# An attention and two-layer feed-forward kernel on one core: value products four slots behind their scores, the first pair normalised in two token halves, the root by Newton steps on VectorE

## The reference, cut to what matters

```python
# q, k, v: (4, 8, 576, 64) float32
rel = pos[:, None] - pos[None, :]
mask = (rel >= 0) & (rel < 64)                  # causal, window of 64
scores = np.where(mask, scale * (q @ k.T), -1e9)
attn = exp(scores - max(scores)); attn = attn / (sum(attn) + 1e-9)
x = (attn @ v), as 2304 tokens x 512

rms = np.sqrt(np.mean(x * x, axis=-1, keepdims=True) + 1e-06)
xn = x / rms * rms_g                            # the normalisation
g = xn @ w_gate; h = g * sigmoid(g) * (xn @ w_val)      # 512 -> 1536
y = h @ w_out                                   # 1536 -> 512
out = (relu(y @ w_in) ** 2) @ w_out2            # 512 -> 2048 -> 512
```

## Time and profile before

| | |
|---|---|
| median of 3 runs | 879.01 us (877.69 to 879.26) |
| the profiled execution, its own time | 876.42 us |
| its span | 874.7 us |
| mean granted TensorE clock | 0.998 of full speed |
| PE busy | 854.7 us (98%) |
| PEld busy | 841.5 us (96%) |
| DVE busy | 591.4 us (68%) |
| ACT busy | 478.8 us (55%) |
| POOL busy | 466.0 us (53%) |

### The profile page before, as it was taken

How to read it: one execution, slowest core, us unless ns; L and a number is a source line. 1 busy time by engine, 2 the same in 40 slices (tenths; PEclk the granted TensorE clock), 3 DMA queues, 4 the chain that set the end, 5 groups by cost and what they waited for, 6 DMA issues and landing times.

```text
span 874.7 us, 16801 instructions
## 1 busy us (share of the span) xinstructions
PE 854.7 (98%) x6388; PEld 841.5 (96%) x6388; DVE 591.4 (68%) x728; ACT 478.8 (55%) x1005; POOL 466.0 (53%) x473
## 2 busy tenths in 40 slices
PE   7798999999999999999999999999999999999998
PEld 5687999999999999999999999999999999999998
DVE  4758675558567548755557767687577787577982
ACT  5887665545565645455555455454555454555451
POOL 3756398683589765388857368400187400386100
PEclk9999999999999999999999999999999999999999
DMA  8863122222222212222212222256632166522687
GB/s 281 263 220 87 49 73 73 61 61 61 84 73 70 70 55 61 79 73 73 73 55 64 81 67 73 56 158 228 218 87 72 56 218 184 176 73 97 182 256 237
DMA packets 107871, 100.18 MB, mean 115 GB/s; under 512 B 6928, under 2 KB 85776, under 8 KB 107792
## 3 DMA queue, kind: packets, MB, share of 16 engines
q1 hardware_dynamic: 92544, 84.14, 32.3%
q10 hardware_dynamic: 15248, 14.98, 4.9%
HBM read 79.69 MB, written 19.40 MB: 113 GB/s over the span
## 4 chain that ended last, share of the span: by engine, by line
PE 90%; DVE 5%; issue 2%; ACT 1%; DMA 1%; POOL 1%; DVEq 0%; ACTq 0%; POOLq 0%
PE banks L844 29%; PE banks L845 28%; PE banks L846 28%; PE banks L803 1%; PE banks L745 1%; DVE probsT L1488 1%; ACT probs L1159 1%; PE banks L817 1%; DMA w_kept<-stash 1%; PE banks L777 1%; DVE acts L1428 0%; DVE banks L1468 0%; DVE d_lo L1574 0%; DVE xc_lo L1460 0%; PE banks L753 0%
## 5 line engine op out<-in xcount | busy, mean ns | idle before, releaser
L844 PE MATMUL banks<-xc_hi,w_hi 128*128 128x384 f32 x844 | 282.6, 335 | 0.2 <-DVE xc_lo L1460 0.2
L846 PE MATMUL banks<-xc_hi,w_lo 128*128 128x384 f32 x844 | 281.9, 334 | 0.0
L845 PE MATMUL banks<-xc_lo,w_hi 128*128 128x384 f32 x844 | 281.9, 334 | 0.0
L844 PE MATMUL banks<-hs_hi,d_hi 128*128 128x384 f32 x544 | 182.4, 335 | 2.3 <-DVE d_lo L1574 2.2
L846 PE MATMUL banks<-hs_hi,d_lo 128*128 128x384 f32 x544 | 181.8, 334 | 0.0
L845 PE MATMUL banks<-hs_lo,d_hi 128*128 128x384 f32 x544 | 181.7, 334 | 0.0
L844 PEld LDWEIGHTS banks<-xc_hi,w_hi 128*128 128x128 f32 x844 | 158.4, 188 | 0.6 <-DVE xc_lo L1460 0.4
L845 PEld LDWEIGHTS banks<-xc_lo,w_hi 128*128 128x128 f32 x844 | 158.4, 188 | 0.0
L846 PEld LDWEIGHTS banks<-xc_hi,w_lo 128*128 128x128 f32 x844 | 158.4, 188 | 0.0
L1405 DVE TENSOR_TENSOR w_lo<-w_raw,w_hi 128x1024 fp32r<-128x1024 f32 x58 | 77.1, 1329 | 81.8 <-ACT w_hi L1090 81.8
L572 POOL TENSOR_TENSOR w_raw<-w_raw 128x256 f32<-128x256 f32 x58 | 60.8, 1047 | 134.0 <-DMA w_raw<-in_w_in 113.6
(11 more groups left out here) (114 smaller groups left out, 1342.5 us busy)
## 6 DMA issues: line engine op xcount, KB each, us to landing
w_kept<-stash SPq DMA_DIRECT2D x56, 256.0 KB, 3.1
w_raw<-in_w_gate SPq DMA_DIRECT2D x36, 256.0 KB, 2.9
w_raw<-in_w_val SPq DMA_DIRECT2D x72, 128.0 KB, 2.8
d_raw<-in_w_out SPq DMA_DIRECT2D x36, 256.0 KB, 2.6
d_raw<-in_w_down SPq DMA_DIRECT2D x32, 256.0 KB, 3.0
v_sb<-in_v_rows SPq DMA_DIRECT2D x16, 384.0 KB, 5.0
w_raw<-in_w_in SPq DMA_DIRECT2D x24, 256.0 KB, 2.7
w_raw<-in_w_in SPq DMA_DIRECT2D x48, 128.0 KB, 2.6
```

The source lines that it names most:

```text
L844: pe.matmul(ps, w_h, v_h, start=first, stop=False, skip_group_check=joined)
L845: pe.matmul(ps, w_h, v_l, start=False, stop=False, skip_group_check=joined)
L846: return pe.matmul(ps, w_l, v_h, start=False, stop=last, skip_group_check=joined)
```

## The change

`PV_LAG` becomes 4: the value products of group `g - 4` stand in slot `g`, and ACT's copies of their results with them. Slot 19 has the products of group 15 and, behind the feed-forward products, those of group 16; slot 20 those of group 17 (`values_in`, `results_in`). On POOL the scaling of the maximum (`biased`) now stands ahead of the add on the sums (`summed`). The first pair is normalised in two chains, one for each half. Per half the four squares are first added in pairs (on POOL in slot 10 for half 0, on DVE in slot 13 for half 1), so PE sums 12 matmuls instead of 24 (slots 11 and 14). The root and the reciprocal are replaced, in all three pairs, by `inverse_root`: a first guess from the bits of the number and two Newton steps, seven small instructions on DVE, each waiting for the one before. ACT takes no root any more.

```diff
-N_LAG, T_LAG, PV_LAG, O_LAG = 1, 2, 3, 3
+N_LAG, T_LAG, PV_LAG = 1, 2, 4
...
+def values_in(g):
+    return [g - PV_LAG] if PV_LAG <= g < TAIL - 1 else [GROUPS - 1] if g == TAIL - 1 else []
+def results_in(g):
+    return [GROUPS - 2, GROUPS - 1] if g == TAIL - 1 else values_in(g)
...
+            def square_two(kh, c):
+                of = x_block(0, kh, c)
+                nc.gpsimd.tensor_tensor(sq_all[:, 2 * kh:2 * kh + 2, c * NT:(c + 1) * NT], of, of,
+                                        ALU.mult).then_inc(sq_pool, 1)
...
                 if g in (8, 9):
                     pool.wait_ge(o_out, O_DONE[A_GROUP + 1])
-                    for k in (2 * (g - 8), 2 * (g - 8) + 1):
-                        square_half(k, 0)
+                    square_two(g - 8, 0)
                 if g == 10:
+                    pool.wait_ge(sq_pool, 2)
+                    nc.gpsimd.tensor_tensor(sq_all[:, 0:2, 0:NT], sq_all[:, 0:2, 0:NT], sq_all[:, 2:4, 0:NT],
+                                            ALU.add).then_inc(sq_added, 1)
+                if g == 11:
+                    first_diagonals(0)
+                if g == 12:
+                    pool.wait_ge(o_out, O_DONE[B_GROUP + 1])
+                    square_two(0, 1)
+                if g == 13:
                     high1_plain(1)
                     high2_plain(1)
-                if g == 13:
-                    diagonals(0)
                 if g == 14:
+                    first_diagonals(1)
+                if g == 15:
                     low1_plain(1)
-                if g == 15:
+                if g == 16:
                     low2_plain(1)
...
-                if g == 10:
+                if g == 11:
                     pe.wait_ge(consts, CONSTS)
-                    pe.wait_ge(sq_pool, KT)
+                    pe.wait_ge(sq_added, 1)
                     first_sums(0, bank[5])
                 if g == 12:
-                    first_sums(1, bank[5])
-                if g == 14:
-                    spread_half(0, bank[5])
+                    spread_half(0, bank[5])
+                if g == 14:
+                    pe.wait_ge(sq_added, 2)
+                    pe.wait_ge(norm_done, KT)
+                    first_sums(1, bank[5])
+                if g == 15:
                     spread_half(1, bank[5])
...
+            def inverse_root(nth, tiles):
+                done = STEPS * nth
+                m, x, e = rms[:, tiles], guess[:, tiles], resid[:, tiles]
+                dve.wait_ge(ms_done, nth + 1)
+                nc.vector.tensor_scalar(x.bitcast(I32), m.bitcast(I32), -0.5, ROOT_SEED, ALU.mult,
+                                        ALU.add).then_inc(rinv_done, 1)
+                for n, (by, plus) in enumerate(ROOT_STEPS):
+                    dve.wait_ge(rinv_done, done + 1 + 3 * n)
+                    nc.vector.tensor_tensor(e, x, x, ALU.mult).then_inc(rinv_done, 1)
...
-                if g == 12:
-                    mean_square(0, bank[5])
-                if g == 13:
-                    inverse(0)
-                if g in (14, 15):
+                if g in (11, 14):
+                    mean_square(nth, bank[5], tiles)
+                    inverse_root(nth, tiles)
+                if g in (12, 13):
...
-                    for k in (2 * (g - 14), 2 * (g - 14) + 1):
+                    for k in (2 * (g - 12), 2 * (g - 12) + 1):
                         normalise(half_cols(0, k, 0), k, bank[5][:, 0:NT])
+                if g == 13:
+                    nc.vector.tensor_tensor(sq_all[:, 0:2, NT:PW], sq_all[:, 0:2, NT:PW], sq_all[:, 2:4, NT:PW],
+                                            ALU.add).then_inc(sq_added, 1)
+                if g in (15, 16):
+                    for k in (2 * (g - 15), 2 * (g - 15) + 1):
+                        normalise(half_cols(0, k, 1), k, bank[5][:, 0:NT])
                 if g in (16, 17):
-                    x_low(0, "B11")
...
+                    x_low(0, ("B11", "B21")[g - 16])
```

More of the change, by code:

```diff
@@ L204, in build @@
         rms = sb("rms", [P, TB], F32)
+        guess = sb("guess", [P, TB], F32)
+        resid = sb("resid", [P, TB], F32)
         assert top[0] <= nc.sbuf_usable_end, (top[0], nc.sbuf_usable_end)
         T1, T2, T3, T4 = [sb(f"T{n + 1}", [P, PW], F32, temp_at + n * PW * 4) for n in range(4)]
-        squares = [[sb(f"sq{n}_{k}", [P, PW], F32, at + k * PW * 4) for k in range(KT)]
-                   for n, at in enumerate((hs_at, h_at + C1 * PW * 4))]
+        sq_all = sb("sq_all", [P, KT, PW], F32, hs_at)
+        squares = [[sq_all[:, k, :] for k in range(KT)],
+                   [sb(f"sq{k}", [P, PW], F32, h_at + (C1 + k) * PW * 4) for k in range(KT)]]
         diag = [sq[0] for sq in squares]
@@ L633, in _ @@
                 if 0 <= n < GROUPS:
+                    total = sums[:, n % PR, :]
+                    pool.wait_ge(exp_done, n + 1)
+                    nc.gpsimd.tensor_scalar(total, total, 1e-9, None, ALU.add).then_inc(summed, 1)
                     pool.wait_ge(inverted, n + 1)
@@ L815, in first_sums @@
                 for n in range(c * TB // 2, (c + 1) * TB // 2):
-                    for k in range(KT):
+                    for k in range(2):
                         mm = pe.matmul(ps[:, n:n + 1], squares[0][k][:, n * P:(n + 1) * P], ones[:, 0:1],
-                                       start=k == 0, stop=k == KT - 1)
-                if c == 1:
-                    mm.then_inc(ms_mm, 1)
+                                       start=k == 0, stop=k == 1)
+                mm.then_inc(ms_mm, 1)
             def spread_part(q, ps, n):
@@ L1162, in _ @@
                     mm.then_inc(exp_done, 1)
-                if g == B_GROUP + O_LAG:
+                if g == B_GROUP + PV_LAG:
                     act.wait_ge(o_out, O_DONE[B_GROUP + 1])
-                    square_half(2, 1)
-                    square_half(3, 1)
-                if g == 12:
-                    root(0)
-                if g in (15, 16):
-                    x_high(0, ("B11", "B21")[g - 15], KT)
+                    nc.scalar.activation(sq_all[:, 2:4, NT:PW], x_block(0, 1, 1), ACT.Square).then_inc(sq_done, 1)
+                if g in (14, 15):
+                    x_high(0, ("B11", "B21")[g - 14], KT)
                 if g in (17, 18):
@@ L1415, in low2, with mean_square @@
                                         ALU.subtract).then_inc(lo2_done, 1)
[L1417 to L1425 removed]
+            def mean_square(nth, ps, tiles):
+                dve.wait_ge(ms_mm, nth + 1)
+                nc.vector.tensor_scalar(rms[:, tiles], ps[:, tiles], 1.0 / D, 1e-6, ALU.mult, ALU.add).then_inc(ms_done, 1)
+            def inverse_root(nth, tiles):
[7 more added lines that the diff above has]
+                    nc.vector.tensor_tensor(e, x, x, ALU.mult).then_inc(rinv_done, 1)
+                    dve.wait_ge(rinv_done, done + 2 + 3 * n)
+                    nc.vector.scalar_tensor_tensor(out=e, in0=e, scalar=by, in1=m, op0=ALU.mult,
+                                                   op1=ALU.mult).then_inc(rinv_done, 1)
+                    dve.wait_ge(rinv_done, done + 3 + 3 * n)
+                    nc.vector.scalar_tensor_tensor(out=x, in0=e, scalar=plus, in1=x, op0=ALU.add,
+                                                   op1=ALU.mult).then_inc(rinv_done, 1)
             def normalise(x, k, by):
```

88 lines of the change are left out of this document (35 added, 53 removed).

## The result

| | before | after |
|---|---|---|
| median of the runs | 878.02 us (14 runs) | 881.75 us (14 runs) |
| the profiled execution, its own time | 876.42 us | 884.91 us |
| its span | 874.7 us | 883.2 us |
| mean granted TensorE clock | 0.998 | 0.986 |

The account below looks back on a forecast made before the run. DVE's slot with its round trip to POOL was taken to set the pace until PE's full stretch; -0.84 for earlier entry, +1.1 value products, +0.75 copy wait gave +1.0 on 879.01, 880.0. Range 875.8 to 883.8.

Parts of the forecast that it names:

- POOL's new order delays DVE by 0.69 us a slot: Attention slots: DVE's reciprocal waits for POOL's `summed` behind `biased`, making DVE's slot 3.31 us instead of 2.62.
- The rival that the order is free: Attention slots: POOL's order costs nothing, ACT bounds at 3.1 us up to group 10, -6.4 us, 873.6; chance 0.08.
- The chains in attention: DVE slots 11 and 14: mean and root, eight dependent instructions, 1.7 us each, 3.4 in all.
- the upper bound I leaned on: DVE's chains: upper bound of the pitch between dependent small instructions, 0.18 + 0.09 = 0.27 us; the lower was 0.13.
- DVE's extras: DVE slots 11 to 17: chains 3.4, normalising two blocks 4.2, add of squares and low part 1.74, together 9.34 us.
- PE's stalls hidden but for 0.3 us: Attention slots: lag 4 gives PE 1.05 to 1.3 us of slack, hiding its waitless stalls but 0.3 us.
- the slower rival: Slots 4 to 10: slack doesn't hide PE's stalls, +3.7 us, 883.7; decides from one stall of about 2 us; chance 0.28.
- Maximum of group 17 at 74.8: Start of DVE's last row maximum: 14.41 + 15 slots x 3.31 + 9.34 + 1.1 + 0.3 = 74.8, against 75.32 before.
- Behind the last maximum: Span after group 17's maximum: forecast 800.9 us, including +1.1 for more value products and +0.75 for ACT's copy.
- In pairs 1 and 2 the chain of seven delays `ga` by about 1.2 us: Later pairs: `va` comes behind it, hidden by two PE products; if not, two pairs lose a few tenths.
- my border of no change: Whole kernel: about 0.2%, 1.8 us, can't be told from no change, so 877.2 to 880.8 counts as same.
- The signs: Attention and after: maxima 3.3 us apart, group 11's at 45 to 46, PE's full stretch at 78.3, no waits behind 87.

Follow-up runs that it names:

- Both repairs together: Changed kernel with POOL's old order and the roots of pairs 1 and 2 at the end of step 8: 874.44 us, 0.9956 of before.
- the roots moved: Changed kernel with the seven small instructions of pairs 1 and 2 moved from the head of step 9 to the end of step 8: 879.07 us.
- after again: The changed kernel run once more, unedited, against the kernel before: 882.04 us, ratio 1.0038.
- the repaired version: Changed kernel, POOL's old order, later roots in step 8, group 16's products between the feed-forward products: 874.30 and 872.80 us; with filler matmuls 873.81.

## Why the prediction was near in time, and which steps failed

The absolute time owes something to luck: 880.0 was +1.0 us on a median of three runs, 879.01, and the kernel before has a median of 878.02 over 14. Measured is +3.4 by medians and +4.2 by the ratio. The sum had these steps; each is held against the runs.

- **POOL's new order delays DVE by 0.69 us a slot: right**, measured 0.7 to 0.8. Of its parts one was sized low: `biased` to `summed` is 0.32, not 0.26, so 15 slots cost 0.9 us more. The rival that the order is free (873.6) fell with the run that restored the old order. Both repairs together took 874.4, near that rival's number, but not by its working: it had 3.1 us a slot up to group 10, and that kernel's profile has 3.6.
- **The chains in attention: right in kind, high in size.** Eight instructions and the next one's start, 1.7 forecast:

```profile
68.24 0.15 DVE L1435 TENSOR_SCALAR rms<-banks 128x3 f32<-128x3 f32 x1
...
69.61 0.17 DVE L1451 SCALAR_TENSOR_TENSOR guess<-resid,guess 128x3 f32<-128x3 f32 x1
69.69 0.69 DVE L1495 COPY_PREDICATED banks<-pick,banks 128x512 f32<-128x512 uint16 x1
```

  1.45 us, at 0.20 apart. Two chains: -0.5. The Trainium skill's rule that the semaphore costs nothing (VectorE: DVE Perf Modes, "The DRAIN you can't avoid"), taken as I took it, would have given 0.13. The rows say 0.03 on top of the duration where an instruction waits for the one before, against 0.08 below it where it doesn't, so they do not bear the rule out, though no run here took the waits out of a chain; the upper bound I leaned on (0.27) was as far off the other way.
- **DVE's extras: right.** Undisturbed slots measured 3.37, with two normalised blocks 4.43, with mean and root on top of one slot's rest 4.84, with blocks and an add 5.29; by my terms 3.31, 4.36, 5.01 and 5.23.
- **PE's stalls hidden but for 0.3 us: too low in all three profiles of this attention stage.** The longest stalls are 2.69, 2.37 and 2.03 us, past the two microseconds from which the slower rival decides (and before itself had 4.7 us of stalls, not the 4.0 that I counted). In the first profile DVE's clock slipped by 1.1, 0.5 and 2.9 us against 3.37 in three slots; in the second by 1.5 and in that of the roots moved by 1.0, both in slot 10, with no other slot from 3 to 9 over 3.69. It varies by execution and it is not part of what the experiments moved. Why PE stands still there, no run shows.
- **Maximum of group 17 at 74.8**: 80.2, 77.1, and 74.9 in three executions of the same attention stage. That the last one meets the forecast is luck: its group 2 was at 13.0 where the sum starts from 14.41. From group 2 to group 17 the three took 65.7, 62.7 and 61.9 us, and the forecast was 60.4; of the difference 0.9 is the pace of 3.37, most of the rest the stalls, less 0.5 for the chains.
- **Behind the last maximum**: 800.9 forecast, 803.0 and 804.0 measured; with the later roots moved 802.4, of which 1.6 is a wait for a DMA. The additional products and the copy (0.85 against my 0.75) are as forecast. What is over is the next step.
- **"In pairs 1 and 2 the chain of seven delays `ga` by about 1.2 us ... I count it as covered": this step failed.** The chain took 3.46 us, not some 1.4, and the rows put that down to POOL at work beside it; `va` came that much later, and PE's two products ahead of it did not cover it. The covering itself was argued rightly: by an estimate from these rows, a chain of 1.4 us, 0.48 to the start of `va` and 0.55 for it end at about 304.7, and PE was ready for it at 305.83 (306.78 less 0.95). It is the chain's price that was wrong. I priced the miss at "a few tenths"; the trace shows 1.9 us of waiting, and moving the chain gave 2.2 to 3.0. That is about the whole of the 2.4 to 3.2 us between forecast (+1.0) and result, and without it the kernel would have been within my border of no change.
- **The signs.** Pace, waits for `sums` and the gap between the last two products (0.85) came as said. Group 11's maximum was to be at 45 to 46: 49.3, 47.1 and 45.3. PE was to enter its full stretch within 2 us of 78.3: it did at 83.8 in the first profile and at 78.5 with the roots moved. PE was to wait nowhere behind 87 us: it does, for `va`. That sign was badly drawn, though: before already waits 2.7 us there, for `d_lo`, a DMA and `xc_lo`, and so the prediction's sentence that PE waits for the last time at 79.17 is wrong.

The account, by ratios, step by step from after to before: POOL's order 4.0 (after again to after with the old order), the later roots 3.2 (from there to both repairs, measured in another batch on another chip), and the rest of the change -3.9: together +3.3, the ratio of after in its batch, as the steps are differences along one line. What stays open is how lag 4's gain and price divide, and why PE's stalls without a wait behind them differ so between executions of one kernel.

## What to carry to other kernels

When two instructions of one queue change places, ask which of them sits in another engine's loop: here a small add between maximum and reciprocal put a round trip of 0.75 us into every slot of the engine that sets the pace, for a wait that had cost little. A chain of small dependent instructions must be priced with its neighbour's work beside it, not from a place where that engine rests, and is better kept from standing ahead of a step that the full engine waits for. And a change with several parts should be timed part by part: here a gain of nearly 4 us was hidden by two costs of about 4 and 3 that two moved blocks of lines take away.

## What the runs showed of the hardware that I had not expected

- A VectorE instruction of 128x6 elements takes 0.17 us beside an idle POOL and 0.59 to 0.98 beside a busy one, and ends within 0.03 us of the POOL instruction's end; this holds for instructions with two inputs and for the one-input TENSOR_SCALAR on integers. A TENSOR_SCALAR of the same size that reads PSUM took 0.16 in the middle of a POOL instruction.
- The granted clock stood at 0.50 from 12 to 20 us, behind an idle time of 2.78 us. Keeping it up with filler matmuls changed the repaired version's time by nothing that could be measured.
- PE's idle time without a wait behind it, in a stretch of many short matmuls, was 4.9 to 5.5 us in each of three executions of the same attention stage, in four pieces, the longest 2.0 to 2.7 us; which slot it lengthened differed.
